# Three-stage kernel, attention and two expert mixtures: gate weights, slot lists, expert choice and warming matmuls reordered

## What is computed

```python
# 1: attention over 7 taps with softmaxed weights, per head of 24 channels
w = exp(weight_gen - max); w = w / (sum(w) + 1e-9)
x = einsum('bshk,bskhg->bshg', w, x_unf)             # x_unf: the 7 rows that end at s
# 2: mixture with two experts of eight per token
noisy = x @ w_gate + log1p(exp(x @ w_noise)) * noise
top2 = the two largest of noisy; weights = softmax over those two
out[token] += weight * (relu(x @ w1[e]) @ w2[e])     # F = 1024
# 3: mixture with one expert of eight per token
xn = x / (norm(x) + 1e-6); en = emb / (norm(emb) + 1e-6)
logits = xn @ en.T / tau; e = argmax(logits)
gate = softmax(logits)[e]
out[token] = gate * (relu(x @ w1[e]) @ w2[e])
```

## Time and profile before

| | |
|---|---|
| median of 3 runs | 1172.62 us (1170.9 to 1174.1) |
| the profiled execution's own time | 1180.06 us |
| its span, first to last instruction | 1178.2 us |
| TensorE matmul busy | 1064.8 us, 90% of the span |
| TensorE weight load busy | 999.5 us, 85% |
| VectorE | 729.1 us, 62% |
| GpSimd | 593.7 us, 50% |
| ScalarE | 525.6 us, 45% |
| mean granted TensorE clock | 0.961 of full speed |

### The profile page before, as it was taken

One profiled execution on the slowest core, in us unless ns is written; L12 is line 12 of the kernel. 1 busy time (PEld: TensorE's weight loads), 2 busy tenths in 40 slices (PEclk: granted clock), 3 DMA queues, 4 the chain that ended last, 5 costly groups with the idle time before them and its releaser, 6 DMA issues.

```text
span 1178.2 us, 27653 instructions
## 1 busy us (share of the span) xinstructions
PE 1064.8 (90%) x7845; PEld 999.5 (85%) x7845; DVE 729.1 (62%) x1473; ACT 525.6 (45%) x1391; POOL 593.7 (50%) x723
## 2 busy tenths in 40 slices
PE   1889347999999999999999999988399999999997
PEld 0566237999999999999999999954199999999997
DVE  8999584556565655656556565556656565567663
ACT  2122253445454544545445454425255454456553
POOL 6888003555555655565555655520034444444443
PEclk9999768999999999999999999989599999999999
DMA  9766793225352352423435334361431331133511
GB/s 332 178 160 166 150 3 87 44 40 103 41 104 39 44 103 40 102 42 47 98 42 100 44 51 92 40 164 39 8 92 41 101 86 56 43 87 111 154 45 32
DMA packets 105846, 98.76 MB, mean 84 GB/s; under 512 B 30899, under 2 KB 96746, under 8 KB 105532
## 3 DMA queue, kind: packets, MB, share of 16 engines
q1 hardware_dynamic: 76412, 62.08, 23.7%
q0 software_dynamic: 29376, 35.97, 18.0%
HBM read 63.82 MB, written 34.98 MB: 84 GB/s over the span
## 4 chain that ended last, share of the span: by engine, by line
PE 82%; DVE 7%; DMA 6%; POOL 3%; issue 2%; ACT 1%; DVEq 0%; POOLq 0%; SPq 0%; ACTq 0%
PE banks L714 23%; PE banks L716 11%; PE banks L700 9%; PE banks L702 7%; PE banks L706 7%; PE banks L701 7%; PE banks L705 7%; DMA token_rows<-gate 3%; PE banks L638 3%; DVE prods L988 3%; POOL prods L475 2%; PE banks L684 2%; PE banks L685 2%; PE banks L619 2%; DMA x_slots<-token_rows,gather_idx 1%
## 5 line engine op out<-in xcount | busy, mean ns | idle before, releaser
L1165 DVE SCALAR_TENSOR_TENSOR h_lo<-banks,h_hi 128x256 fp32r<-128x256 f32 x736 | 312.1, 424 | 336.4 <-ACT h_hi L891 297.5
L891 ACT ACTIVATE h_hi<-banks 128x256 fp32r<-128x256 f32 x736 | 282.7, 384 | 419.6 <-PE banks L706 386.9
L714 PE MATMUL banks<-w_hl,h_hi 128*128 128x384 f32 x1472 | 465.8, 353 | 0.0
L716 PE MATMUL banks<-w_hl,h_lo 128*128 128x192 f32 x1472 | 367.5, 250 | 0.0
L716 PEld LDWEIGHTS banks<-w_hl,h_lo 128*128 128x128 f32 x1472 | 279.4, 190 | 0.0
L714 PEld LDWEIGHTS banks<-w_hl,h_hi 128*128 128x128 f32 x1472 | 276.7, 188 | 0.2
L487 POOL DMA_INDIRECT x_slots<-token_rows,gather_idx x188 | 188.9, 1005 | 112.2 <-POOL gather_idx L480 81.7
L506 POOL DMA_INDIRECT token_rows<-y_slots,store_idx x120 | 193.6, 1614 | 84.7 <-issue 58.0
L700 PE MATMUL banks<-x_hi_a,w_hi 128*128 (+1 forms) x736 | 226.7, 308 | 0.0
L706 PE MATMUL banks<-x_hl_b,w_lo 128*128 (+1 forms) x736 | 207.4, 282 | 0.0
L701 PE MATMUL banks<-x_hi_a,w_lo 128*128 (+1 forms) x736 | 207.3, 282 | 0.0
(11 more groups left out here) (177 smaller groups left out, 1156.1 us busy)
## 6 DMA issues: line engine op xcount, KB each, us to landing
raw<-in_moe_w SPq DMA_DIRECT2D x17, 768.0 KB
token_rows<-stage SPq DMA_DIRECT2D x28, 384.0 KB, 5.1
raw<-in_moe_w SPq DMA_DIRECT2D x17, 512.0 KB
raw<-in_moe_w SPq DMA_DIRECT2D x34, 256.0 KB
token_rows<-zeros SPq DMA_DIRECT2D x14, 386.0 KB, 6.9
x_halo<-in_x SPq DMA_DIRECT2D x2, 2688.0 KB, 15.3
rows<-token_rows SPq DMA_DIRECT2D x14, 384.0 KB, 7.3
x_slots<-token_rows,gather_idx POOLq DMA_INDIRECT x188
```

The source lines that it names most:

```text
L714: mm(y[:, i, 0:2 * D], h_hi[:, c % HBUFS, t], w2_hl[u][:, c, :, :], start=c == 0, stop=False)
L716: ins = mm(y[:, i, 0:D], h_lo[:, c % HBUFS, t], w2_hl[u][:, c, 0, :], start=False, stop=c == FC - 1)
L891: sc.activation(h_hi[:, c % HBUFS, :], banks[:, c % HBANKS, 0:BLOCK], ACT.Relu).then_inc(h_hi_ready[m], 1)
L1165: v.scalar_tensor_tensor(h_lo[:, c % HBUFS, :], banks[:, c % HBANKS, 0:BLOCK], 0.0, h_hi[:, c % HBUFS, :].bitcast(F32), ALU.max, ALU.subtr ...
```

## The change

Four edits.

- `finish_gates()` is called right behind the running sum (L1050), ahead of the block totals, and no longer ahead of one-hot group 1.
- The four decoding operations run twice, for columns 0 to 7 and for the rest. `ids_ready` = 1 is signalled after the first part. Since `turn_slots` writes into bank 3, from which the second part still reads, TensorE waits for `ids_ready` = 2 ahead of the first turn.
- `keep_clock(10)` ahead of each mixture becomes 22 matmuls for m = 0 and 14 for m = 1.
- For m = 1, `pick(0, scores)` runs twice, for groups 0 to 10 as soon as their scores are there and for groups 11 to 13 after the last. The subtraction of the best score moves from `weigh_best` into these two parts.

```diff
@@ -28,6 +28,7 @@
 GROUP = 4
 HI_FROM, LO_FROM = 2, 4
 EMB_AT = 6
+EARLY_GROUPS = 11
 TURN_AT = 2
 Y_AT = 1
 X_SPLIT_AT = 4
@@ -39,7 +40,8 @@
 ONEHOTS = 8
 PAIR = 2
 QUAD = 4
-GATES_AT = 1
+FIRST_COLS = 8
+WARM = (22, 14)
 HOT_BUFS = 3
 PAD_ROW = 1 << 16
 CODE_MIN = 71 * 128
@@ -686,9 +688,10 @@
                     ins.then_inc(x_turned[m], 1)
 
                 pe.sem_inc(h_used[m], HBUFS)
-                keep_clock(10)
+                keep_clock(WARM[m])
                 pe.wait_ge(table_ready[m], 1)
                 ends = expert_ends(pe, m)
+                pe.wait_ge(ids_ready[m], 2)
                 pe.wait_ge(gathered[m], 16 * HALVES)
                 turn_slots(0)
                 keep_clock(4)
@@ -1026,14 +1029,16 @@
             v.memset(cum[:, 0:1], 0.0)
             step(v.memset(block_end[:, 0:1], 0.0))
 
-            def pick(k, scores):
-
-                step(v.tensor_reduce(best[k][:], scores[:], AX.X, ALU.max))
-                step(v.tensor_tensor(r["tie"][:], scores[:], best[k][:].unsqueeze(2).to_broadcast([P, T, E]), ALU.is_equal))
-                ranks = expert_rank[:].unsqueeze(1).to_broadcast([P, T, E])
-                step(v.tensor_tensor(r["tie"][:], r["tie"][:], ranks, ALU.mult))
-                step(v.tensor_reduce(rank[:], r["tie"][:], AX.X, ALU.max))
-                step(v.tensor_tensor(onehot[k][:], ranks, rank[:].unsqueeze(2).to_broadcast([P, T, E]), ALU.is_equal))
+            def pick(k, scores, at=slice(0, T)):
+
+                shape = [P, at.stop - at.start, E]
+                tie, top = r["tie"][:, at, :], best[k][:, at]
+                step(v.tensor_reduce(top, scores[:, at, :], AX.X, ALU.max))
+                step(v.tensor_tensor(tie, scores[:, at, :], top.unsqueeze(2).to_broadcast(shape), ALU.is_equal))
+                ranks = expert_rank[:].unsqueeze(1).to_broadcast(shape)
+                step(v.tensor_tensor(tie, tie, ranks, ALU.mult))
+                step(v.tensor_reduce(rank[:, at], tie, AX.X, ALU.max))
+                step(v.tensor_tensor(onehot[k][:, at, :], ranks, rank[:, at].unsqueeze(2).to_broadcast(shape), ALU.is_equal))
 
             def positions(m, weigh, finish_gates):
 
@@ -1048,6 +1053,7 @@
                 flat = counts[:].rearrange("p e t -> p (e t)")
 
                 step(v.tensor_tensor_scan(cum[:, 1:], flat, flat, 0.0, ALU.add, ALU.max))
+                finish_gates()
                 first_of_expert, last_of_expert = cum[:, 0:E * T:T], cum[:, T::T]
                 step(v.tensor_tensor(totals[:], last_of_expert, first_of_expert, ALU.subtract))
 
@@ -1085,8 +1091,6 @@
                 for g in range(n // ONEHOTS):
                     if g >= HOT_BUFS:
                         dve.wait_ge(hots_used[m], g - HOT_BUFS + 1)
-                    if g == GATES_AT:
-                        finish_gates()
                     tiles = slice(g * ONEHOTS, (g + 1) * ONEHOTS)
                     for k, width, done in (("hi", cols, hi_hots_ready), ("lo", P, hots_ready)):
                         shape = [P, ONEHOTS // PAIR, width, PAIR]
@@ -1096,13 +1100,18 @@
                 block_table()
                 v.memset(gather_rows[:, cols:cols + AHEAD], 0)
                 dve.wait_ge(hots_used[m], n // ONEHOTS)
+                for at in (slice(0, FIRST_COLS), slice(FIRST_COLS, cols)):
+                    q = {k: a[:, at] for k, a in (*idf.items(), *idi.items())}
+                    step(v.tensor_tensor(quad_codes[:, at, :], banks[:, 2:2 + QUAD, at].rearrange("p i c -> p c i"),
+                                         quad_scale[:].unsqueeze(1).to_broadcast([P, at.stop - at.start, QUAD]), ALU.mult))
+                    step(v.tensor_reduce(q["id_bits"], quad_codes[:, at, :], AX.X, ALU.max))
+                    step(v.tensor_scalar(q["id_code"], q["id_bits"].bitcast(I32), 16, None, ALU.logical_shift_right))
+                    ins = v.tensor_scalar(gather_rows[:, at], q["id_code"], float(-CODE_MIN), 0.0, ALU.add, ALU.max)
+                    if at.start == 0:
+                        ins.then_inc(ids_ready[m], 1)
+                    else:
+                        step(ins)
                 q = {k: a[:, 0:cols] for k, a in (*idf.items(), *idi.items())}
-                step(v.tensor_tensor(quad_codes[:, 0:cols, :], banks[:, 2:2 + QUAD, 0:cols].rearrange("p i c -> p c i"),
-                                     quad_scale[:].unsqueeze(1).to_broadcast([P, cols, QUAD]), ALU.mult))
-                step(v.tensor_reduce(q["id_bits"], quad_codes[:, 0:cols, :], AX.X, ALU.max))
-                step(v.tensor_scalar(q["id_code"], q["id_bits"].bitcast(I32), 16, None, ALU.logical_shift_right))
-                v.tensor_scalar(gather_rows[:, 0:cols], q["id_code"], float(-CODE_MIN), 0.0, ALU.add, ALU.max).then_inc(ids_ready[m], 1)
-                dve.wait_ge(ids_ready[m], 1)
                 if CHOICES[m] == 2:
                     step(v.tensor_scalar(q["id_second"], gather_rows[:, 0:cols], N - 0.5, float(N), ALU.is_gt, ALU.mult))
                     step(v.tensor_tensor(q["id_row"], gather_rows[:, 0:cols], q["id_second"], ALU.subtract))
@@ -1210,15 +1219,18 @@
                 step(v.tensor_tensor(square[:], rows[:, tiles, :], rows[:, tiles, :], ALU.mult))
                 v.tensor_reduce(sumsq[:, tiles], square[:], AX.X, ALU.add).then_inc(norms_ready, 1)
 
-            dve.wait_ge(logits_ready[1], NG)
             scores = logits[:, :, 0:E]
-            pick(0, scores)
+            for first, last in ((0, EARLY_GROUPS), (EARLY_GROUPS, NG)):
+                dve.wait_ge(logits_ready[1], last)
+                tiles = slice(first * GROUP, last * GROUP)
+                pick(0, scores, tiles)
+                step(v.tensor_tensor(r["noisy"][:, tiles, :], scores[:, tiles, :],
+                                     best[0][:, tiles].unsqueeze(2).to_broadcast([P, (last - first) * GROUP, E]), ALU.subtract))
 
             def weigh_best():
                 dve.wait_ge(roots_ready, 1)
                 step(v.tensor_scalar(inv_norm[:], inv_norm[:], 1e-6, None, ALU.add))
                 step(v.reciprocal(inv_norm[:], inv_norm[:]))
-                step(v.tensor_tensor(r["noisy"][:], scores, best[0][:].unsqueeze(2).to_broadcast([P, T, E]), ALU.subtract))
                 v.tensor_tensor(r["noisy"][:], r["noisy"][:], inv_norm[:].unsqueeze(2).to_broadcast([P, T, E]),
                                 ALU.mult).then_inc(route_ask[1], 1)
```

## The result

The changed kernel takes **1164.46 us** (median of 6 runs, 1163.49 to 1165.86), the kernel before in the same session 1173.01 us (6 runs, 1170.9 to 1174.1). The ratio is 0.9929, 95% interval 0.9916 to 0.9942. So it is faster by 8.5 us and not by 14.5; the time lies just above the range given. The profiled execution took 1164.12 us (span 1162.3), where that of before took 1180.06. In what follows, "before" stands for the kernel before.

The account below looks back on a forecast made before the run. Gapless TensorE mixtures start late, waiting for the gates' store behind the token rows, then the slot list. Gains of 7.2 and 7.3 us, together 14.5, off the 1172.6 us median gave 1158.1 us, range 1154.0 to 1164.0.

Parts of the forecast that it names:

- the sum's last line: Whole kernel: the 14.5 us gain, worked out on the profiled 1180.06 us, subtracted from the median 1172.6, giving 1158.1 us.
- step 4: Ahead of each mixture: more warming matmuls keep TensorE's clock high for the first turn, gaining 0.45 us in each.
- step 5: Start of each mixture: GpSimd's copy and gathers run beside VectorE's second list part, costing 0.2 us each.
- rival A: Start of both mixtures: gates' store stays last, taking 2 to 3 us more in one or both; 1160 to 1162 us, chance 0.11.
- Gates behind the sum: First mixture: store's transfer starts at 145.29 and lands 24.85 us later at 170.14, leaving the list last by 0.9 us.
- List in two parts: Both mixtures: gathers start on the first 8 columns, decoded in 0.81 us; first copy at 171.18, 6.9 us gained.
- Pick in two parts: Ahead of the second mixture: most picking done in idle time, 2.19 us earlier for all that follows; copy 7.1 us earlier.
- Warming: TensorE ahead of the mixtures: 22 matmuls take 5.1 us, 14 at most 5.9; high clock gains 0.45 us each.
- The new neighbour: GpSimd's copy and gathers beside VectorE's second list part: slowed by 0 to 1.0 us, taken as 0.2 us per mixture.
- B: Rival, TensorE ahead of the mixtures: warming overshoots at a low clock, first turn 3.2 us late; 1162.2 us, chance 0.10.
- C: Rival, ScalarE ahead of the first mixture: program load queued behind the earlier store delays activations; 1177 us, chance 0.02.
- D: Rival, mixtures: the early start is given back, one stretch gaining nothing through an unseen wait; 1165 us, chance 0.05.

Follow-up runs that it names:

- before_c: The kernel before, unchanged, profiled once more in a further session: 1172.91 us, ratio 1.0002; its profiled execution took 1173.74 us.
- gates_late: The changed kernel with the gates' operations put back ahead of one-hot group 1, the other three edits kept: 1175.36 us, ratio to before 0.9986.
- before_again: The kernel before, unchanged, profiled a second time in a further session: 1176.57 us, ratio 1.0002; its profiled execution took 1176.14 us.

## Why the prediction was wrong

**The step that failed is the sum's last line:** "The median is 7.4 us lower than it, in stretches that the change doesn't touch or that I can't place, and I take the gain as absolute". Nearly all of it, 6.5 us, was in the two stores, the very waits that the change takes away. The gain was worked out against an execution in which they took 37.5 us and subtracted from a median whose executions have about 31 (this figure is that of `before_c`, a session with the same median; no trace shows the stores in the three timed executions themselves, and the changed kernel's trace has 31.5). With the stores of the execution of 1173.74 us the same working gives 2.0 us in the first mixture (19.92 + 0.17 us from the store's start to the copy, against 171.18 - 153.10 = 18.1), and 26.02 - 20.52 = 5.5 in the second (from pick to copy, 842.42 - 816.40). With the two turns' 0.9 (step 4) and without the 0.4 of step 5 that is 8.4 us, 1164.2; measured were 8.5 and 1164.46. Left on the slow execution the sum would have said 1165.6 for the changed kernel, which no longer waits for the stores: 1.1 us off.

The same slip is in rival A. It asked whether the store could be *slower* later; it did not ask whether it is *faster* in most executions. And the agreement of the two stores (24.85 and 2 x 12.64), given there as proof of a fixed pace, only shows that the pace holds within one execution.

**Step by step**, the trace of the changed kernel against the forecast:
- Gates behind the sum: right. The transfer starts near 145.3, and the list and not the store is last. Its landing after 24.85 and 12.64 us: wrong, 20.0 and 11.5.
- List in two parts: right. First copy at 171.06 (171.2 forecast), last step of the list ends at 174.28 (174.3). TensorE's new wait never showed.
- Pick in two parts: right. Six operations from 812.49 to 814.20, pick to copy 20.50 us (20.52).
- Warming: it took 4.91 and 5.58 us (5.1 and at most 5.9), and ended 0.2 us ahead of the second turn. The turn is fast, as forecast, 0.69 us from the first transpose to the gate copy. But its cause was the shorter wait: ten matmuls do as well for the turn, so the reason was wrong, and that the number came right was luck. The caution that the slow matmuls' number differs from run to run was borne out (4.63 us for the same 14 in the other session), with no cost.
- The new neighbour: wrong in sign. GpSimd's copy took 0.19 us, its gathers 1.20 and 0.96, and the way from copy to turn was 4.78 us, 0.26 *less* than before. Before, with VectorE idle beside them, the same two gathers took 1.20 and 0.96 too. VectorE paid: one 120-wide operation beside the first gather took 0.49 us, the next of that width 0.22. The list's last step came 0.3 us later for it, covered by the 1.6 us (175.84 - 174.28) left ahead of the turn. The held operation had begun at 172.28, 0.74 us after the gather, and ended at 172.77, right behind the gather's 172.74. In `gates_late`, where the gather comes only at 176.34, the same operation took 0.22 us, so the gather is the cause. The prediction had given the wait to the wrong engine.
  The Trainium skill ("SBUF — State Buffer", Who interferes with whom) states that a `tensor_scalar` of VectorE in a mode with two ports and an instruction of GpSimd exclude each other, and that whoever issues first has the shared ports for its whole instruction. The trace agrees for the end of the gather and not for its whole length: in the second mixture, beside a gather from 833.45 to 834.49, two `tensor_scalar` took the 0.20 us that they take in `gates_late` without one, and only the third, which met the gather's end, was held (0.29 against 0.20, ending at 834.49). No run shows in which mode they ran.

VectorE and GpSimd of the changed kernel in order of time, VectorE's last two rows from the second mixture:

```profile
172.28 0.49 DVE L1108 TENSOR_SCALAR id_code<-id_bits 128x120 int32<-128x120 int32 x1
172.80 0.22 DVE L1109 TENSOR_SCALAR gather_rows<-id_code 128x120 int32<-128x120 int32 x1
...
833.74 0.20 DVE L1108 TENSOR_SCALAR id_code<-id_bits 128x64 int32<-128x64 int32 x1
...
834.20 0.29 DVE L1120 TENSOR_SCALAR id_part<-gather_rows 128x72 int32<-128x72 int32 x1
...
171.54 1.20 POOL L489 DMA_INDIRECT x_slots<-token_rows,gather_idx  x1 [0.30 <-POOL gather_idx L482]
```

The first of these operations in `gates_late`, with no gather beside it:

```profile
172.50 0.22 DVE L1109 TENSOR_SCALAR id_code<-id_bits 128x120 int32<-128x120 int32 x1
```

- The mixtures stay gapless, rivals B, C and D did not occur: the warming did not overshoot, ScalarE's 28 activations show no gap, and nothing was given back.

**What stays open.** Why the store's pace differs between sessions wasn't found: eleven traces from the sessions with a before near 1176 us have 21.9 to 22.8 us for the pair, the two from sessions near 1173 us have 19.9 and 20.0. Each later session ran on another chip (14, 1, 5 and 9 near 1176 us, 3 near 1173), and none on one chip twice, so it isn't shown whether the pace belongs to the chip or to the moment. It isn't shown either why the one profiled execution of before had 24.85 us; one of the twelve timed runs of `before_again` took 1180.2 us, but its stores are on no trace. The gates' move alone wasn't seen beside a before of 1173 us.

## What to carry to other kernels

Where a profiled execution is longer than the median, the excess has a place, and until it is found the stretch that a change removes is a candidate for it: work the gain out with the excess outside it and inside it, and let the range hold both (here 14.5 and 14.5 - 7.4 = 7.1 us; measured 8.5). A DMA of many tiny pieces is the first suspect. And a change that hides such a transfer gains a different amount in each session; its own time is the steadier number.

## What the runs showed that was not expected

- 14,336 four-byte pieces took 19.9 to 24.9 us and 7,168 took 11.0 to 12.7, by session and execution. In before itself, three executions gave 24.85, 21.88 and 19.92 us for the pair. The traces of one later session agreed to 1 us.
- TensorE kept its full clock over 3.3 us without work (ten warming matmuls, then the turn at 0.30 us for a transpose), and had lost it after 5.6 us (22 matmuls, then 0.45 us for a transpose). Between the two the length of the wait doesn't tell: in the three executions with the gates' move alone, waits of 4.3 to 4.4 us ahead of the first turn were followed by a first transpose of 0.33 us, but in two of them the clock fell inside the turn (0.42 us for the last); and one wait of 2.5 us ahead of the second turn was enough to find it falling (0.38, then 0.42 us).
